# mLSTM, MLP and mixture of experts in one program: exponents of the first two chunks by row halves, a chunk's sums and state in four places, weights through SyncE's queue

## The reference, cut to what matters

```python
# 1: mLSTM, 2 batches, 8 heads, 768 positions, head dimension 40; for each position t
m_new = max(f[t] + m, i[t]); f_stab = exp(f[t] + m - m_new); i_stab = exp(i[t] - m_new)
C = f_stab * C + i_stab * outer(v[t], k[t]);  n = f_stab * n + i_stab * k[t]
y[t] = sigmoid(o[t]) * (C @ q[t]) / max(abs(n . q[t]), 1)
# 2: MLP on 1536 tokens of 320:  h = x @ w_in (320 x 2048);  x = (h - tanh(h)) @ w_out
# 3: four experts:  out += p[:, e] * (relu(x @ w1[e]) @ w2[e])   (320 x 1024 x 320)
```

## Time and profile before

| | us |
|---|---|
| runs of before, median (lowest to highest) | 609.2 (608.38 to 609.33) |
| the profiled execution | 609.59 |
| its span, first to last instruction | 607.8 |
| TensorE busy | 597.1 (98%) |
| VectorE, ScalarE, GpSimd busy | 236.7, 195.2, 117.9 |
| mean granted clock of TensorE | 0.994 |

### The profile page before, as it was taken

One profiled execution on the slowest core, in us unless ns is written; L12 is line 12 of the kernel. 1 busy time (PEld: TensorE's weight loads), 2 busy tenths in 40 slices (PEclk: granted clock), 3 DMA queues, 4 the chain that ended last, 5 costly groups with the idle time before them and its releaser, 6 DMA issues.

```text
span 607.8 us, 8875 instructions
## 1 busy us (share of the span) xinstructions
PE 597.1 (98%) x3689; PEld 542.6 (89%) x3689; DVE 236.7 (39%) x474; ACT 195.2 (32%) x389; POOL 117.9 (19%) x100
## 2 busy tenths in 40 slices
PE   8989899999999999999999999999999999999998
PEld 7888899998888899999999999999999999999997
DVE  6466575665654554331323223231323132313232
ACT  4655553435334255541112321113311111111111
POOL 3895511110100007750002520003400000000000
PEclk9799999999999999999999999999999999999999
DMA  6964522230300002440000220001000000001011
GB/s 240 328 239 179 198 103 103 103 103 1 103 1 1 1 0 96 143 139 5 1 1 0 96 96 1 1 0 49 1 1 0 2 1 0 1 1 43 1 43 44
DMA packets 10629, 37.51 MB, mean 62 GB/s; under 512 B 1294, under 2 KB 3166, under 8 KB 10590
## 3 DMA queue, kind: packets, MB, share of 16 engines
q1 hardware_dynamic: 7134, 19.65, 9.0%
q0 software_dynamic: 3456, 17.30, 8.2%
HBM read 34.92 MB, written 2.02 MB: 61 GB/s over the span
## 4 chain that ended last, share of the span: by engine, by line
PE 91%; DMA 3%; DVE 3%; issue 1%; ACT 1%; SPq 0%; POOL 0%; DVEq 0%; ACTq 0%
PE bank L908 11%; PE bank L909 11%; PE bank L910 11%; PE bank L956 9%; PE bank L957 9%; PE bank L958 9%; PE bank L911 5%; PE bank L912 5%; PE bank L929 4%; PE bank L931 3%; PE bank L930 3%; PE bank L795 3%; DMA w_raw<-in_w 3%; PE bank L785 2%; PE bank L935 2%; PE bank L936 2%
## 5 line engine op out<-in xcount | busy, mean ns | idle before, releaser
L762 DVE SCALAR_TENSOR_TENSOR g_lo<-bank,g_hi 128x512 fp32r<-128x512 f32 x96 | 66.4, 692 | 253.5 <-ACT g_hi L546 253.5
L546 ACT ACTIVATE g_hi<-bank 128x512 fp32r<-128x512 f32 x96 | 57.4, 598 | 269.9 <-PE bank L912 269.9
L908 PE MATMUL bank<-x_hi,w_all 128*128 128x512 f32 (+2 forms) x318 | 118.4, 372 | 1.0 <-DVE x_hi L675 0.9
L956 PE MATMUL bank<-w_all,g_hi 128*128 128x320 f32 x384 | 118.6, 309 | 0.0
L958 PE MATMUL bank<-w_all,g_lo 128*128 128x320 f32 x384 | 118.3, 308 | 0.0
L957 PE MATMUL bank<-w_all,g_hi 128*128 128x320 f32 x384 | 118.2, 308 | 0.0
L909 PE MATMUL bank<-x_lo,w_all 128*128 128x512 f32 (+2 forms) x318 | 118.0, 371 | 0.0
L910 PE MATMUL bank<-x_hi,w_all 128*128 128x512 f32 (+2 forms) x318 | 117.7, 370 | 0.0
L381 POOL TENSOR_TENSOR w_all<-w_raw,w_all 128x1408 fp32r<-128x1408 f32 x16 | 51.6, 3224 | 217.4 <-ACT w_all L453 217.4
L956 PEld LDWEIGHTS bank<-w_all,g_hi 128*128 128x128 f32 x384 | 72.0, 188 | 3.7
L957 PEld LDWEIGHTS bank<-w_all,g_hi 128*128 128x128 f32 x384 | 72.1, 188 | 3.5
(11 more groups left out here) (118 smaller groups left out, 691.2 us busy)
## 6 DMA issues: line engine op xcount, KB each, us to landing
w_raw<-in_w POOLq DMA_DIRECT2D x24, 704.0 KB, 4.4
feat<-in_feat SPq DMA_DIRECT2D x12, 512.0 KB, 5.6
tok<-in_tok SPq DMA_DIRECT2D x12, 484.0 KB, 6.7
zb<-z SPq DMA_DIRECT2D x10, 512.0 KB, 4.5
out<-arena SPq DMA_DIRECT2D x12, 160.0 KB, 1.9
g_tmp<-in_gates SPq DMA_DIRECT2D x1, 64.0 KB
z<-zr SPq DMA_DIRECT2D x1, 56.0 KB, 6.8
g_tmp<-in_gates SPq DMA_DIRECT2D x1, 48.0 KB
```

Of the source, the lines that this page charges most:

```text
L546: A(g_hi[:, b, 0:N], h_ps[b][:, 0:N], ACT.Relu).then_inc(ghi_ready, 1)
L762: V.scalar_tensor_tensor(g_lo[:, b, 0:N], h_ps[b][:, 0:N], 0.0, g_hi[:, b, 0:N].bitcast(F32), ALU.max, ALU.subtract).then_inc(g_ready, 1)
L908: mm(h, up_part(m, 0, k), x_hi[:, k, c], start=k == 0, stop=False)
L956: mm(out, g_hi[:, b, t], high_w, start=first, stop=False)
```

## The change

For chunks 0 and 1 the exponents are built together, chunk 0 in rows 0 to 63 of the array and chunk 1 in rows 64 to 127, matmul by matmul in turn. The decays are computed behind the first products, the first values are weighed by VectorE straight from PSUM, and the copy of the weights wa comes in step 0; the first states move from step 0 to step 1. Pieces of weights are issued by SyncE, in its one queue. ScalarE's high split of pieces 0 to 7 is in two operations in two places. A chunk's row sums start behind the first of two products. VectorE's work on sums and state of a chunk, one run at k = 2 before, is in four places: sums and rows, then the state's product, behind `inter` at k = 2 (both in `finish_sums`); the gate before g_lo at k = 3 (`gate_rows`); the state's addition behind g_lo at k = 3 (`finish_state`, from another bank). Starts of chunks 2, 3 and 4 are 3, 7 and 10 instead of 2, 6 and 11.

```diff
+START = {2: 3, 3: 7, 4: 10, 5: 15, 6: 19, 7: 23, 8: 27, 9: 34, 10: 38, 11: 42}
 SUMS, TURN = 2, 4
...
-        split_at = {0: -1, 1: -1, 2: 0, 3: 3, 4: 4, 5: 7, 6: 9, 7: 12}
+        split_at = {0: -1, 1: -1, 2: 1, 3: 4, 4: 5, 5: 8, 6: 9, 7: 11}
...
+            def load_piece(k):
+                if k >= RING:
+                    sp.wait_ge(w_ready, k - RING + 1)
+                sp.dma_start(w_raw[:, k % RING, :], w_d[k, :, :]).then_inc(raw_in[k % RING], 16)
...
             load_tok(1)
+            load_piece(0)
+            load_piece(1)
             sp.wait_ge(z_rows, 1)
             sp.dma_start(z_d, zr[:, :]).then_inc(z_out, 16)
+            load_piece(2)
             sp.wait_ge(z_out, 16)
             load_z(2)
-            load_z(3)
-            sp.wait_ge(tok_in[1], 16)
             load_feat(2)
             load_tok(2)
+            load_z(3)
             sp.dma_start(probs[:, :, :], probs_d).then_inc(probs_in, 16)
+            load_piece(3)
+            load_piece(4)
+            behind = {3: (5, 6), 4: (7,), 5: (8,), 6: (9,), 7: (10,)}
             for n in range(RING, STEPS):
...
                     load_z(n + 1)
+                for k in behind.get(n, ()):
+                    load_piece(k)
+            for k in range(11, PIECES):
+                load_piece(k)
...
                                     ALU.subtract).then_inc(w_ready, 1)
-                if k + RING < PIECES:
-                    pool.wait_ge(w_ready, k + 1)
-                    load_piece(k + RING)
...
-            pool.wait_ge(gboth_high, 1)
-            load_piece(0)
-            load_piece(1)
             for n in range(BATCH):
                 for q in range(2):
                     cut_first(n, q)
-            pool.wait_ge(raw_in[1], 16)
-            load_piece(2)
             split_low(0)
-            weigh_v(0)
-            weigh_v(1)
+            split_low(1)
             cut_z(2)
-            split_low(1)
             split_low(2)
             weigh_v(2)
             cut_z(3)
@@ -428,8 +430,8 @@
             cut_z(4)
             split_low(5)
             split_low(6)
+            weigh_v(4)
             cut_z(5)
-            weigh_v(4)
             split_low(7)
             for n in range(5, STEPS):
                 if n + 1 < STEPS:
...
                 w, raw = w_all[:, k % WARM, :], w_raw[:, k % RING, :]
                 if k < WARM:
                     A(w[:, 0:DN0 + D], raw[:, 0:DN0 + D], ACT.Copy)
-                    A(w[:, DN0 + SIDE:DN0 + SIDE + D], raw[:, DN0 + D:PIECE], ACT.Copy).then_inc(whi_ready, 1)
                 else:
                     A(w[:, 0:PIECE], raw, ACT.Copy).then_inc(whi_ready, 1)
+            def split_rest(k):
+                w, raw = w_all[:, k % WARM, :], w_raw[:, k % RING, :]
+                A(w[:, DN0 + SIDE:DN0 + SIDE + D], raw[:, DN0 + D:PIECE], ACT.Copy).then_inc(whi_ready, 1)
             def first_exps(n, q, bank_):
-                act.wait_ge(e_ready, 2 * n + q + 1)
+                act.wait_ge(e_ready, 2 * q + n + 1)
                 after(act, p_done, 2 * n + q - 1)
...
             split_high(0)
+            split_rest(0)
+            x_high(0, c_ps)
             split_high(1)
-            x_high(0, c_ps)
-            act.wait_ge(weigh_t, 1)
-            A(wa[:, :, :], bank[4][:, 0:3 * ROWS].rearrange("p (k r) -> p k r", r=ROWS), ACT.Copy).then_inc(wa_ready, 1)
             x_high(1, up_ps[0])
+            split_rest(1)
...
+                    if m == 0:
+                        act.wait_ge(wv_ready, BATCH)
+                        A(wa[:, :, :], bank[4][:, 0:3 * ROWS].rearrange("p (k r) -> p k r", r=ROWS),
+                          ACT.Copy).then_inc(wa_ready, 1)
                     for n, k in phase(m):
                         if k == TURN:
                             x_high(n, c_ps)
+                        if k == 1:
+                            gate(n)
+                    for k in range(2, WARM):
+                        if split_at[k] == m - 1:
+                            split_rest(k)
...
@@ -539,8 +555,6 @@
                     for n, k in phase(m):
                         if k < 1:
                             exps_by_head(n, k + 1)
-                        if k == 1:
-                            gate(n)
...
-            lows(g_both, gr)
+            low_rows(g_both, gr, 0)
             dve.wait_ge(top_ready, 1)
             dve.wait_ge(tboth_high, 1)
-            lows(t_both, top)
+            low_rows(t_both, top, 0)
+            low_rows(g_both, gr, 64)
+            low_rows(t_both, top, 64)
...
+            tops = bank[4][:, 0:P]
...
+            def decays():
                 chain.done(V.tensor_tensor(high[:, 0:ROWS], before[:, 0:ROWS], tops[:, 0:ROWS], ALU.max))
...
@@ -622,8 +642,12 @@
                 chain.wait()
                 chain.done(V.reciprocal(dn[:, :], dn[:, :]))
                 chain.wait()
+                chain.done(V.tensor_tensor(y, y, spread(dn[:, :], HD), ALU.mult))
+            def gate_rows(n, o_ps):
+                y = heads(o_ps[:, 0:HEADS * HDE])[:, :, 0:HD]
                 o = tok[:, n % RING, 2 * D + HEADS:3 * D + HEADS].rearrange("p (h d) -> p h d", d=HD)
-                chain.done(V.tensor_tensor(y, y, spread(dn[:, :], HD), ALU.mult))
                 chain.wait()
                 after(dve, t_ready, n - 1)
                 dve.wait_ge(eo_ready, n + 1)
...
...
+                gate_rows(n, o_ps)
+            def weigh_first(n):
+                r = row0(n)
+                V.tensor_tensor(wv[:, n, :, :], tok[:, n, D:2 * D + HEADS].rearrange("p (h e) -> p h e", e=HDE),
+                                spread(bank[4][:, r:r + HEADS], HDE), ALU.mult).then_inc(wv_ready, 1)
+            def first_states():
                 dve.wait_ge(sums_ready, BATCH)
                 for half in range(2):
...
+                    V.tensor_copy(state[part, :, half::2, :], c_ps[part, 0:BATCH * PAIRS * HDE].rearrange(
+                        "p (n j e) -> p n j e", n=BATCH, e=HDE)).then_inc(state_ready, 1)
             def finish_sums(n):
                 r0, own = row0(n), state[0:KP, n % 2, :, :]
-                dve.wait_ge(sums_ready, n + 1)
+                dve.wait_ge(inter_ready, n - 1)
                 after(dve, y_ready, n)
                 chain.done(V.tensor_tensor(num, heads(a_ps[:, 0:HEADS * HDE]),
                                            spread(wa[:, 1, r0:r0 + HEADS], HDE), ALU.mult))
+                chain.wait()
+                chain.done(V.tensor_tensor(heads(c_ps[:, 0:HEADS * HDE]), num, heads(c_ps[:, 0:HEADS * HDE]), ALU.add))
+                chain.wait()
+                rows_out(n, c_ps)
                 dve.wait_ge(beta_ready, 1)
                 dve.wait_ge(state_ready, n)
                 chain.done(V.tensor_tensor(own, own, spread(beta[0:KP, r0:r0 + HEADS], HDE), ALU.mult))
-                chain.wait()
-                V.tensor_tensor(heads(c_ps[:, 0:HEADS * HDE]), num, heads(c_ps[:, 0:HEADS * HDE]),
-                                ALU.add).then_inc(o_ready, 1)
+            def finish_state(n):
+                dve.wait_ge(sums_ready, n + 1)
+                chain.wait()
                 for half in range(2):
                     part = slice(64 * half, 64 * half + HD)
                     mine = state[part, n % 2, half::2, :]
-                    last = V.tensor_tensor(mine, mine, heads(a_ps[part, HEADS * HDE:HEADS * HDE + PAIRS * HDE]), ALU.add)
+                    last = V.tensor_tensor(mine, mine, heads(b_ps[part, 0:PAIRS * HDE]), ALU.add)
                 last.then_inc(state_ready, 1)
-            def finish_rows(n):
-                dve.wait_ge(o_ready, n - 1)
-                rows_out(n, c_ps)
...
+            decays()
             scores(1, 0, bank[0])
             scores(1, 1, bank[1])
             first_rows(0, c_ps)
             first_rows(1, up_ps[0])
+            dve.wait_ge(weigh_t, 1)
+            weigh_first(0)
             x_low(0, c_ps)
             x_low(1, up_ps[0])
+            weigh_first(1)
...
+                        if k == SUMS + 1:
+                            gate_rows(n, c_ps)
...
                         if k == SUMS:
                             finish_sums(n)
-                            finish_rows(n)
-                    if m == 0:
-                        first_state(0)
-                        first_state(1)
+                        if k == SUMS + 1:
+                            finish_state(n)
+                    if m == 1:
+                        first_states()
...
-                pe.wait_ge(p_done, 2 * n + 2)
                 pe.wait_ge(tok_in[r], 16 * (n // RING + 1))
-                for h in range(HEADS):
-                    last = mm(o_ps[:, h * HDE:(h + 1) * HDE],
-                              pwork[:, n % 2, h % 2, (h // 2) * CH:(h // 2 + 1) * CH],
-                              tok[:, r, D + h * HDE:D + (h + 1) * HDE], start=True, stop=True)
+                for q in range(2):
+                    pe.wait_ge(p_done, 2 * n + q + 1)
```

(33 more changed lines are left out.)

28 lines of the change are left out of this document (9 added, 19 removed).

## The result

The changed kernel took 599.9 us (median of four, 598.93 to 601.56), the kernel before 609.27: a ratio of 0.9849, 95% interval 0.9819 to 0.988, so 9.4 us less where 6.9 were forecast. A second set of executions of the same changed kernel (e9) has a median of 601.22 and a ratio of 0.9851, 0.9831 to 0.987.

The account below looks back on a forecast made before the run. TensorE, busy 98%, bounds the kernel; its 533.0 us from step 16 carry over. Step 0 at 18.35 plus stretch 49.5 (45.7 + 1.75 + 2.0) puts step 16 at 67.9, 6.9 earlier: span 600.9, time 602.3 us, range 598.8 to 606.4.

Parts of the forecast that it names:

- The sum: Steps 0 to 16 added: step 0 at 18.35, stretch 49.5, step 16 at 67.9, 6.9 us earlier; 602.3 us.
- rival A: More gain: the low clock ends sooner or never comes and the hand's waits are covered; 599.0 to 600.5 us, chance 0.17.
- the forecast's low stage: Clock 0.50 from about 15 us, assumed to stay low until the same 21.7 us as before.
- the clock term: Steps 0 and 1 run while the clock is low: 1.75 us lost instead of 0.8.
- the term for waits: TensorE's waits left in steps 0 to 16: 1.3 us placed plus 0.7 unseen of the same kind, 2.0 in all.
- the front: Everything ahead of step 0: step 0 at 18.35 us, 1.9 earlier, with bounds 0 to 2.4.
- Rival C: The front gives nothing: row halves don't overlap, exponents 2.9 us, step 0 at 20.2; 604.2 us, chance 0.08.
- The forecasts of the queue: SyncE's one queue: z by 15.7 us behind two pieces, feat of later chunks behind waits for w_ready, cost nothing.
- the late piece 2: POOL issued weights piece 2 at 15.80, landing at 24.03; SyncE would bring it by 17.5 us.
- a price of 0.9 wherever it recurs: VectorE's state product in a chunk's sums: 1.59 us stays possible where it took 0.7 elsewhere.
- Rival B: Waits come back between tanh and g_lo, 1.1 us a chunk on average, 3.3 in all; 605.6 us, chance 0.19.
- Rival D: Slower: the low clock stays, past 21.7 by more than 14 us; 609.4 us and more, chance 0.03.

Follow-up runs that it names:

- e2: Changed kernel, but exponents of chunks 0 and 1 one behind the other over the full array, chunk 0's scores between them; 600.45 us, ratio 0.9848 to before.
- e6: Kernel before, with only the weight pieces issued by SyncE in the new order; 606.94 us, ratio 0.9958 to before.
- e1: Changed kernel, but with POOL issuing the weight pieces again, in the places where it did before; 603.76 us, ratio 0.9892 to before.
- e7: Kernel before, with only VectorE's four places, started by the end of inter, and the new state in its own bank; 606.61 us, ratio 0.9949.
- e4: Changed kernel, but with the state's addition and the gate in one run with sums and rows again; 603.01 us, ratio 0.9891 to before.
- e5: Changed kernel, but with old starts 2, 6, 11 and also the old steps for the weight pieces' high splits; 602.87 us, ratio 0.9884 to before.
- e3: Changed kernel, but with chunks 2, 3 and 4 starting in steps 2, 6 and 11 as before; 608.39 us, ratio 0.9983 to before.
- e11: Changed kernel, but with row sums that wait for both products of a chunk; 602.26 us, ratio 0.986 to before.
- e10: Changed kernel, but with ScalarE's high split of pieces 2 to 7 in one place again; 600.35 us, ratio 0.9835 to before.
- e12: Kernel before, with both weights issued by SyncE and VectorE's four places; 603.48 us, ratio 0.989 to before.
- e8: Changed kernel, with 6 more 512-column matmuls that only keep TensorE busy ahead of step 0; 601.64 us, ratio 0.9873 to before.

## Why the prediction was right, and where it was not

*Where the time could come from.* Right: everything behind step 16 was carried over to 0.05 us, and all of the gain lies ahead.

*The point and the rival.* The sum said 602.3, the result was 599.9, inside the range, but not in the forecast's own part of it (600.5 to 604): it is what rival A (the low clock shorter or gone, waits covered) put at 599.0 to 600.5. The median of e9, the same kernel, is 601.22 and lies in the forecast's part; which of the two four executions give is luck. The runs show that A is not an alternative but a share of executions: at 1.000 the change gives 597.2, with the forecast's low stage 599.1 to 599.8, which is 600.85 to 601.56 in time. So of the 2.4 us between forecast and median about 1.3 are the clock term, and 1.1 is the sum itself. One of its signs failed with it: step 16 was to begin at 67 to 69, by the sum at 67.9, and began at 64.13. Of the 3.8 us, 1.75 are the clock term, 1.0 the term for waits and 0.9 the front (half of that the piece from the last transposition to step 0, 1.33 us at full clock for the 1.85 of the sum, which came from rows at the low one).

*The term for waits was too large.* 2.0 us of waits were left in the sum. The bare sum 45.7 against the measured 46.68 leaves 1.0. The 0.7 put on top for waits "of the same kind" was not there, and the wait of chunk 4's scores for the state was 0.3, not 0.6.

*Exponents.* The halves overlap, as forecast: 1.7 forecast for both chunks, 1.35 measured, under the lower bound of 1.44. The two of 512 columns take 0.3 together (6.86 to the first small one at 7.15), and the eight small ones 0.40 us, to the next pair at 7.55, so 0.05 each and not the 0.07 of L785. Rival C falls with this, and e2 shows that the halves are worth 1.5 us at full clock, 0.7 at 0.997. C's sign alone, step 0 at 20, would have misled: e9 has it at 20.38 with halves that overlap.

*The front under a low clock was missed.* The sum took over the fall at 15 us. Where the fall comes at 12.3 (e9) it slows the row sums as well, and step 0 stands at 20.38, not 18.35. That e9's step 16 at 67.69 agrees with the forecast's 67.9 is no support for the parts: the front was 2.0 too early, the stretch 2.2 too long (49.5 against 47.31).

*Weights by SyncE.* The forecasts of the queue held: z readable at 15.57 (15.7), feat of chunk 3 behind a wait, without cost. The reason given for the gain, the late piece 2, is confirmed only in small part: in the old kernel e6 shows 0.35 us less wait at step 2's down, and the larger part of the shorter stretch is the wait for yt, behind a state product that met a shorter operation of POOL. In the new one the loss without it (e1) came through tok of chunk 0, which the prediction had on no path; what a late piece 2 costs there is open.

*Sums and state in four places.* The mechanism was right (waits for g_lo and for yt behind a chunk go). The whole of it is worth 2.7 us in the old plan (e7); in the new one the addition and the gate alone are worth 1.2 to 1.5 (e4). The slow state product, which the forecast gave a price of 0.9 wherever it recurs, is there once in after's stretch (1.17 at 58.32 instead of 0.49), and TensorE's waits show at most 0.2 us behind it. The forecast named POOL's splits beside it only as a risk; the traces show that the product ends about 0.36 us behind POOL's operation.

*Starts.* Right that the wait of step 16 for x_hi goes: e5 has it back with 0.9 us. The prediction gave the steps of the splits no word, as it priced only the kernel in which both moved; e3's expectation treated the starts as an edit of their own, and was wrong by the 3.7 us of the mismatch (52.15 against 47.65, 0.8 of the difference clock). *Row sums in halves* were to begin 0.65 earlier for each chunk; e11 shows one wait of 0.17 in the stretch without them, and 0.64 in the front.

*ScalarE's split* was given a gain in words; e10 shows none.

*Rival B* (waits come back between tanh and g_lo, 3.3 us) did not happen: 0.5 us of waits for g_lo in two places, the largest 0.3. *Rival D* (slower by a clock that stays low) did not either, though the low stage reached step 0 in e9.

What stays open: what sets the moment of the clock's fall, what moves before by up to 2.7 us at one mean clock, and what of the last 1 us or so between e12 and after belongs to the weighings on VectorE and to the first states one step later.

## What to carry to other kernels

Read first from where on the bound engine has no waits, carry that part over unchanged, and price the change only ahead of it: this part was right to 0.05 us, and the errors were all in the rest. In a hand-written schedule the step of a chunk's work and the step of the work that feeds it are one edit; moving one alone cost here 3.7 us of 9. Where a kernel has a light stretch in which the clock may fall, sort the executions by mean clock before reading a difference of 1 or 2 us: medians of four differed from the equal-clock comparison by 1 us one way (e2) and by 1.6 to 3 the other (e4, e1). And when an edit helps, look which wait went: e6 helped, mostly by a wait that its theory did not name.

## What the runs showed of the hardware

- The mean clock of an execution and its span go together in the changed kernel: 597.2 us at 1.000, 598.4 at 0.997, 599.1 to 599.8 at 0.994, 600.7 at 0.991; the same program, unchanged, shows all four. In the kernel before the medians of 0.997 and 0.994 differ by 1.2 us too (607.4 and 608.65), but single executions do not follow: 609.2 at 1.000, and 606.6 to 609.3 at 0.994.
- Matmuls of 64 rows in the two halves of the array, two of 512 and eight of 128 columns in turn, took 0.69 us a round (6.86 to 7.55). In the trace of before, one of 512 and four of 128 over all rows took the same 0.69 (from 6.86 to 7.55): the second chunk was free.
- One queue with everything in order brought tok of chunk 0 at 10.4 to 11.3 us (after, e9, e4, e8); with the weight pieces on POOL's queue beside it, it came at 12.3 (e1), and tok of chunk 1 at 13.6 to 15.2 (before, e7, e1) instead of 12.2 to 12.5 (e9, e4, e6, e8). From 8.5 to 14 us 405 GB/s were moved in after and 377 in e1, so the order of service is the likelier cause than the rate; it was not tried by itself.
- VectorE's product of the state and its decay (104 x 328, both operands in SBUF) took 0.49 us wherever no operation of POOL was running at its start. In 20 places of the 14 profiles one was; there the product took 0.57 to 2.08 us and ended 0.35 to 0.37 us behind POOL's operation, whether that was a split, a cut of z or a weighing (before 36.45, after 58.32, e6 34.57, e10 49.59; in e7 at 65.74 behind a second one that followed at once). Only in e12 at 63.69, where POOL had less than 0.1 us left, it took 0.49. What it costs depends on the path: with 1.58 us in before TensorE waited 0.9 for yt, with 1.25 and 1.32 in e10 the stretch is as long as after's.
